# Loading k, q and v of a batch head by head: four transfers over 128 partitions in place of transfers over 64

## The reference

```python
# q, k, v: (8 batches, 8 heads, 576, 64) float32;  p: (8, 8, 32, 64)
def sm_attn(qq, kk, vv):                       # softmax attention, scale 1/8
    s = scale * np.matmul(qq, kk.transpose(0, 1, 3, 2))
    a = np.exp(s - np.max(s, axis=-1, keepdims=True))
    a = a / (np.sum(a, axis=-1, keepdims=True) + 1e-09)
    return np.matmul(a, vv)
p_packed = sm_attn(p, k, v)                    # 32 rows attend over k, v
out = sm_attn(q, p_packed, p_packed)           # 576 queries attend over the 32 packed rows
x = out.transpose(0, 2, 1, 3).reshape(4608, 512)
h = x @ w_in                                   # 512 -> 1024
solu = h * softmax(h)
ln = (solu - mean) / sqrt(var + 1e-06) * g_ln
y = ln @ w_out                                 # 1024 -> 512
h2 = max(y @ w1, y @ w2, y @ w3)               # 512 -> 768
result = h2 @ w_out2                           # 768 -> 512
```

## Time and profile before

| | |
|---|---|
| runs | 1096.96, 1093.41, 1096.2 us; median 1096.2 |
| profiled execution | 1094.8 us, of which the instructions span 1093.2 us |
| PE busy | 1030.2 us, 94% of the span |
| DVE, ACT, POOL busy | 606.3, 345.6 and 250.8 us |
| granted TensorE clock, mean | 0.978 of full |
| moved by DMA | 183.23 MB, mean 168 GB/s |

### The profile page before, as it was taken

The page is one execution under the profiler, slowest core; times in us unless marked ns, Lnnn a source line. Parts: engine busy times, 40 slices in busy tenths (PEclk is TensorE's granted clock), DMA queues, the critical chain, the costliest instruction groups (busy, mean ns, idle before and its releaser), DMA issues.

```text
span 1093.2 us, 15814 instructions
## 1 busy us (share of the span) xinstructions
PE 1030.2 (94%) x6498; PEld 815.8 (75%) x6498; DVE 606.3 (55%) x980; ACT 345.6 (32%) x551; POOL 250.8 (23%) x222
## 2 busy tenths in 40 slices
PE   5778868799999999999999999999999999999998
PEld 4444534487888888888888888888888888888887
DVE  1367757767657747765646653667355563654021
ACT  3345544333423414432422233222322142222111
POOL 0112354448398439832000000000000000000000
PEclk9789989899999999999999999999999999999999
DMA  9988985234366145511575444554455535543251
GB/s 201 247 214 205 250 216 148 100 138 156 118 233 227 65 156 179 223 44 77 212 279 188 176 166 162 183 179 179 154 186 176 185 137 191 177 156 112 98 171 39
DMA packets 47144, 183.23 MB, mean 168 GB/s; under 512 B 8032, under 2 KB 8032, under 8 KB 37472
## 3 DMA queue, kind: packets, MB, share of 16 engines
q1 hardware_dynamic: 40848, 147.21, 42.6%
q0 software_dynamic: 6224, 35.00, 8.7%
HBM read 134.62 MB, written 47.58 MB: 167 GB/s over the span
## 4 chain that ended last, share of the span: by engine, by line
PE 78%; DVE 9%; DMA 5%; issue 4%; ACT 2%; POOL 1%; SPq 1%; ACTq 0%
PE ps L1088 27%; PE ps L723 24%; PE ps L1120 13%; PE ps L1111 4%; PE ps L737 2%; PE ps L988 2%; DMA q_raw<-in_q_dram 2%; PE ps L870 2%; DMA w_in_s<-in_moe_w_in_dram 2%; DVE a2T L1570 1%; DMA k_raw<-in_k_dram 1%; DVE h_lo L1479 1%; DVE spot L1776 1%; PE ps L828 1%; DVE spot L1767 1%
## 5 line engine op out<-in xcount | busy, mean ns | idle before, releaser
L1088 PE MATMUL ps<-ys,slot 128*128 128x512 f32 x1512 | 345.8, 390 | 0.5
L1088 PEld LDWEIGHTS ps<-ys,slot 128*128 128x128 f32 x1512 | 283.3, 188 | 62.4 <-ACT spot L1163 3.9
L1767 DVE TENSOR_TENSOR spot<-ps,spot 128x512 f32<-128x512 f32 x108 | 74.3, 688 | 99.7 <-PE ps L1088 74.2
L1163 ACT ACTIVATE spot<-ps 128x512 f32<-128x512 f32 x90 | 52.8, 596 | 207.5 <-PE ps L1088 196.4
L723 PE MATMUL ps<-ln_hi,w_out_s_lo 128*128 128x512 f32 x280 | 109.1, 390 | 0.0
L723 PE MATMUL ps<-ln_hi,w_out_s_hi 128*128 128x512 f32 x280 | 109.0, 389 | 0.0
L723 PE MATMUL ps<-ln_lo,w_out_s_hi 128*128 128x512 f32 x280 | 109.0, 389 | 0.0
L1120 PE MATMUL ps<-w_out_s_lo,h_hi 128*128 128x512 f32 x216 | 84.1, 389 | 0.0
L1120 PE MATMUL ps<-w_out_s_hi,h_lo 128*128 128x512 f32 x216 | 84.1, 389 | 0.0
L1120 PE MATMUL ps<-w_out_s_hi,h_hi 128*128 128x512 f32 x216 | 84.1, 389 | 0.0
L1294 ACT ACTIVATE u<-ps,neg_max 128x1024 f32<-128x1024 f32 x36 | 40.2, 1117 | 124.0 <-DVE neg_max L1645 124.0
(11 more groups left out here) (152 smaller groups left out, 1500.9 us busy)
## 6 DMA issues: line engine op xcount, KB each, us to landing
slot<-w_operands SPq DMA_DIRECT2D x36, 1792.0 KB, 7.3
w_operands<-stage POOLq DMA_DIRECT2D x18, 1024.0 KB, 4.9
k_raw<-in_k_dram SPq DMA_DIRECT2D x32, 288.0 KB, 5.9
v_raw<-in_v_dram SPq DMA_DIRECT2D x16, 576.0 KB, 9.4
q_raw<-in_q_dram SPq DMA_DIRECT2D x16, 576.0 KB
y_features<-yst SPq DMA_DIRECT2D x9, 1024.0 KB, 4.4
y_raw<-y_features SPq DMA_DIRECT2D x9, 1024.0 KB, 5.6
out_dram<-spot SPq DMA_DIRECT2D x36, 256.0 KB, 2.1
```

The lines of the kernel that those rows point to most:

```text
L1088: last = pe.matmul(ps[:, group_bank(g, k), :], w[:, a - 1, i, kk, :], ys[:, b, j, kk, :], start=n < 4 and kk == 0 and e == 0, stop=kk == K ...
L1163: return act.activation(dst, src, ACT.Copy)
L1767: dve.tensor_tensor(dst[:, :], a, b, op).then_inc(ready, 1)
```

## The change

All three inputs are viewed with the head ahead of the quad, and a load becomes four transfers, one for each head h of a quad. Each fetches head h of both quads: its destination is `k_raw[:, h, :, :]` (likewise `v_raw`, `q_raw`), all 128 partitions with 2304 bytes in each, and its source is `k_v[b, h]`, which has the dimensions quad (2), row (64), 576 numbers. Before, a transfer of v or q fetched the four heads of one quad into 64 partitions, and one of k two of those heads. k keeps its two semaphores, with the same heads behind each. v and q now count to 64 for each batch. The waits, the order of the loads on SP and everything else are as they were.

```diff
     def rows(t):
-        return t.rearrange("b (g h) (p j) d -> b g p h (j d)", g=QUADS, j=J)
+        return t.rearrange("b (g h) (p j) d -> b h g p (j d)", g=QUADS, j=J)
...
-                for x in range(2):
-                    for g in range(QUADS):
-                        sp.dma_start(k_raw[half(g), 2 * x:2 * x + 2, :, :].rearrange("p h j d -> p h (j d)"),
-                                     k_v[b, g][:, 2 * x:2 * x + 2, :]).then_inc(k_loaded[x], 16)
+                for h in range(QH):
+                    sp.dma_start(k_raw[:, h, :, :].rearrange("p j d -> p (j d)"), k_v[b, h]).then_inc(k_loaded[h // 2], 16)
...
-                for g in range(QUADS):
-                    sp.dma_start(v_raw[half(g), :, :, :].rearrange("p h j d -> p h (j d)"), v_v[b, g])\
-                        .then_inc(v_loaded, 16)
+                for h in range(QH):
+                    sp.dma_start(v_raw[:, h, :, :].rearrange("p j d -> p (j d)"), v_v[b, h]).then_inc(v_loaded, 16)
...
-                for g in range(QUADS):
-                    sp.dma_start(q_raw[half(g), :, :, :].rearrange("p h j d -> p h (j d)"), q_v[b, g])\
-                        .then_inc(q_loaded, 16)
+                for h in range(QH):
+                    sp.dma_start(q_raw[:, h, :, :].rearrange("p j d -> p (j d)"), q_v[b, h]).then_inc(q_loaded, 16)
...
-                    pe.wait_ge(q_loaded, 32 * b + 32)
+                    pe.wait_ge(q_loaded, 64 * b + 64)
...
-                pe.wait_ge(v_loaded, 32 * b + 32)
+                pe.wait_ge(v_loaded, 64 * b + 64)
```

## The result

The changed kernel takes 1496.45 us (median of four runs, 1495.55 to 1497.64) against 1096.26 us (1093.41 to 1096.96): a ratio of 1.366, 95% interval 1.3631 to 1.3685. It is 400 us slower. The forecast was 1535 us, with a range of 1470 to 1690.

A forecast was written before the change was run, and what follows sets the result against it. Transfers were taken to bound the attention part (first 186 us), PE the 908 us behind. Last q at 581 + 39 + 3 = 623 us, 437.5 later; 1094.8 + 437.5 + 2 = 1534, so 1535 us forecast, range 1470 to 1690.

The forecast's parts named there:

- Where the change acts: Only the first 186 us, up to the last q's landing, change; the 908 us behind keep their length.
- the 2 us that the sum adds behind the last q: Last term of the forecast sum: 2 us added to 1094.8 + 437.5.
- Two engines: Loads of k, v, q: source's outermost count of 2 puts each transfer on two DMA engines; last q at 623 us.
- The price of a byte: Each new k, v or q transfer takes 6.05 us on its two engines; 96 of them take 581 us.
- The rest: Up to the last q: 39 us for the two engines' other bytes and small packets, 3 us for start and last landing.
- The queue never dry: Attention part: the two engines are never idle and alone set the pace; a batch brings 77.5 us of load.
- The rival on the other side: Loads dealt by 128 destination rows over sixteen engines: 7.0 us a batch freed, 30 us gained, 1065 us; chance 0.08.
- Why the loads were slow before: Loads of k, q, v covering 64 partitions move 228 GB/s, against 407 for w_in over 128; half the partitions is slow.

The follow-up runs named there:

- e3: Changed kernel with neighbouring heads on the two quads (head 2h+g in place of 4g+h), so a source's 128 rows are one run: 1080.6 us, ratio 0.9854.
- e7: On top of e3, w_in issued right behind the first q and p loaded by eight transfers of 32 partitions: 1076.2 us, ratio 0.9817.
- e1: Kernel before the change with only q loaded in the new form, k and v as before: 1253.5 us, ratio 1.1425.
- e2: Changed kernel with each transfer cut in two, one for each quad (64 partitions, source outermost 64): 1091.1 us, ratio 0.9939.

## Why the prediction was right, and where it was off

*Where the change acts.* Right. The cut at the last q held: 906 us behind it against 908. No run shows the 2 us that the sum adds behind the last q: that stretch was 2 us shorter, not longer, with a granted clock of 0.50 from 588 to 592 us and of 0.97 from 592 to 600.

*Two engines.* Right, and the step on which everything rested. The closing packets fell to exactly the numbers written down (7200 and 40,016), the share of 0.13 says two engines as well, and the cut at the quad, which changes the source's outermost count from 2 to 64 and leaves head order and bytes alone, gave all the time back; e3 kept the 128 partitions and did too. In e3 a source of 4 x 32 x 64 had four engines. So three counts (2, 4, and 32 or more) were seen, with 2, 4 and 16 engines (7200, 8464 and 9360 packets under 512 bytes, each as counted ahead). Which engines they are (the expectation of e7 names 0 to 3 for p), and what counts other than these do, no run shows.

*The price of a byte.* This term was mis-sized. I took 6.05 us a transfer, between w_in's 25.4 GB/s and the store's 23.4; it took 5.60 (26.3 GB/s). Both rows were taken with sixteen engines at work, and a lone pair went a little faster than the fastest of them. Why, no run separates. That a lone pair wouldn't crowd as sixteen engines on 64 partitions do was an estimate when I wrote it; the runs show 26.3 GB/s for each of the pair, and 14.1 for each of the sixteen in the kernel before. 96 x 0.45 is 43 us, against a forecast that was 39 us too high.

*The rest.* I had 42 us beside k, v and q (39 and 3). The last q's landing leaves 588.0 - 96 x 5.60 = 50 us. Which of its parts was short (the stores, p's small packets, or w_in and w_out on the two engines) no run separates.

*The queue never dry.* Right: SP issues without a gap and a step is 73.2 us (77.5 forecast). What I had not seen is that SP no longer waits at its semaphores (3.0 us in place of 120): it stands in its issues. The e1 run shows the limit of the argument: with only q slow the two engines do run dry between one q and the next, and there the sum of the loads came out at least 23 us too low.

*The rival on the other side.* That the 128 destination rows decide the deal is ruled out: the new transfers have them and were dealt over two engines (7200 packets). Sixteen engines over 128 partitions is what e3 makes real, and it is worth 16 us, not 30. I had taken PE's load waits and the stalls within `pack` together as the gain. Two thirds of them stayed: 8.9 us in `pack`, 12.1 us for k and q; and the wait for w_in rose from 2.1 to 8.1 us. By the waits alone that is 6 us. Most of the rest is PE itself: up to the last q it was busy 128.2 us in place of 138.0 for the same matrix products, with a granted clock of 0.92 in place of 0.90 (a matmul of the q and k turns took 307 ns on average in place of 327). As I read it, less waiting left less work at the lower clock behind the waits (0.50 in the 4 us behind the changed kernel's last wait for q); the rival had no term for that.

*Why the loads were slow before.* The prediction put it down to the half of the partitions that a transfer covered. The numbers agree in part: 228 against 407 GB/s, and e3 with its 128 partitions moves 239 GB/s at a share of 0.75 in place of 218 at 0.91. But e2, with 64 partitions in each transfer, moves its 218 at 0.74, so the half alone doesn't tell a slow transfer from a fast one, and what made the loads slow no run shows. The change had a sound aim and lost it to the shape of the source.

## What to carry to other kernels

Before a transfer is reshaped, write down the outermost count of both sides as the instruction will carry them: a count of 2 or 4 on the DRAM side left 2 or 4 DMA engines at work here, and widening the SBUF side to 128 partitions was worth nothing where the DRAM side started with a 2 (1496 us in place of 1096). Count closing packets (small packets less the pieces that are small themselves) to see the number of engines, as every trace here allowed; a low mean DMA share beside long waits for loads (0.19 and 412.5 us up to the last q here) is the other sign. Where two blocks can't be joined in DRAM, relabel which blocks go together, as the neighbouring heads do, rather than let one transfer step over the gap.

## What the runs showed that I had not expected

SP's issue blocks. With 64 rows for each of two engines, the first two transfers were issued in 0.70 and 0.56 us, the third and fourth in 4.55 and 5.23. Everything behind on SP stands too, a p transfer for all sixteen engines among it: the one at 11.95 us took 5.58 us to issue. It is not a matter of two engines alone: in e3 the four issues of p at 35 us took 11.50 us in all, with w_in and k in the queue.

Cutting at the quad was faster than the kernel before by 0.6% (interval 0.4 to 0.9%), although SP issues 24 transfers a batch in place of 8. Up to the last q its DMA engines are less busy for what they move (columns as in the earlier trace rows):

```profile
0.00:186.00 186.00, 136.00 (x2397) 81.88 (x2398) 102.60 (x195) 80.65 (x155) 52.38 (x49) 0.88 0.74 218
```

That is 218 GB/s over 16 x 0.74 engines, 18.4 GB/s for a busy one, where the kernel before has 15.0 (218 over 16 x 0.91). These rates are rough, since the share goes above 1 in the earlier trace rows. The execution behind this view took 1095.46 us, the slowest of the six, and its span (1093.8 us) is that of the kernel before (1093.2): it shows emptier engines, but not where the 0.6% came from. Its transfers alternate between the two halves of the partitions every 147 KB instead of every 295 or 590. Whether that is what leaves them emptier, no run here shows.
